# Gates of the second unit moved off GpSimd, last turns copied by ScalarE, one rounding in another form, and a new order

## The reference

```
mag = sqrt(a_re**2 + a_im**2); scale = min(mag, 0.999) / (mag + 1e-6)
ar, ai = a_re * scale, a_im * scale
S_re, S_im = ar*S_re - ai*S_im + outer(k, v), ar*S_im + ai*S_re
y[t] = q[t] @ S_re
```

## Time and profile before

| | |
|---|---|
| median of 3 runs | 913.99 us (913.25 to 916.9) |
| profiled execution, its own time | 915.01 us |
| its span | 913.3 us |
| mean granted TensorE clock | 0.987 |
| TensorE busy | 842.6 us, 92% |
| VectorE busy | 446.1 us, 49% |
| ScalarE busy | 490.1 us, 54% |
| GpSimd busy | 334.9 us, 37% |

### The profile page before, as it was taken

The page is one execution under the profiler, slowest core; times in us unless marked ns, Lnnn a source line. Parts: engine busy times, 40 slices in busy tenths (PEclk is TensorE's granted clock), DMA queues, the critical chain, the costliest instruction groups (busy, mean ns, idle before and its releaser), DMA issues.

```text
span 913.3 us, 14419 instructions
## 1 busy us (share of the span) xinstructions
PE 842.6 (92%) x5692; PEld 729.8 (80%) x5692; DVE 446.1 (49%) x628; ACT 490.1 (54%) x737; POOL 334.9 (37%) x254
## 2 busy tenths in 40 slices
PE   0168889889999999999999999999999999999997
PEld 0158889878887888788888888888888889898986
DVE  5689886848585848484848422333121121212020
ACT  7669778585959586868695535642121211211121
POOL 1165734534444444344444323556122221303120
PEclk9988999999999999999999999999999999999999
DMA  7664262444444443444352433021010101000000
GB/s 296 150 224 133 58 207 80 152 136 128 111 119 141 124 122 108 142 123 123 107 159 71 141 135 144 0 67 55 18 53 9 61 1 70 1 35 1 36 0 35
DMA packets 71011, 88.45 MB, mean 97 GB/s; under 512 B 15392, under 2 KB 55840, under 8 KB 70432
## 3 DMA queue, kind: packets, MB, share of 16 engines
q1 hardware_dynamic: 70944, 87.53, 30.8%
HBM read 59.13 MB, written 28.39 MB: 96 GB/s over the span
## 4 chain that ended last, share of the span: by engine, by line
PE 56%; issue 3%; POOL 1%; POOLq 0%; DVE 0%; ACT 0%
PE bank L1243 55%; POOL hl L593 1%; PE bank L1258 0%; POOLq L114 0%; DVE xl L947 0%; ACT osb L704 0%; POOLq L690 0%
## 5 line engine op out<-in xcount | busy, mean ns | idle before, releaser
L593 POOL TENSOR_TENSOR gl<-ge,gh 128x512 fp32r<-128x512 f32 x96 | 131.2, 1367 | 190.4 <-ACT gh L704 190.4
L947 DVE TENSOR_TENSOR hm<-bank,hm 128x512 f32<-128x512 f32 x72 | 49.8, 692 | 226.6 <-PE bank L1243 224.7
L1243 PE MATMUL bank<-xh,wih 128*128 128x512 f32 (+1 forms) x336 | 125.8, 374 | 6.9 <-DVE ge L944 3.6
L944 DVE SCALAR_TENSOR_TENSOR ge<-ge,bank 128x512 f32<-128x512 f32 x96 | 65.8, 685 | 130.9 <-ACT ge L704 130.9
L1243 PE MATMUL bank<-xh,wal 128*128 128x512 f32 x324 | 126.1, 389 | 0.0
L1243 PE MATMUL bank<-xl,wah 128*128 128x512 f32 x324 | 126.1, 389 | 0.0
L1243 PE MATMUL bank<-xh,wah 128*128 128x512 f32 x324 | 126.0, 389 | 0.0
L1243 PE MATMUL bank<-gh,woh 128*128 128x512 f32 (+1 forms) x336 | 124.1, 369 | 0.2
L1243 PE MATMUL bank<-xh,wil 128*128 128x512 f32 (+1 forms) x336 | 122.0, 363 | 0.0
L593 POOL TENSOR_TENSOR hl<-hm,hh 128x512 fp32r<-128x512 f32 x36 | 46.5, 1293 | 205.8 <-ACT hh L704 205.8
L1243 PE MATMUL bank<-xl,wih 128*128 128x512 f32 (+1 forms) x336 | 121.8, 363 | 0.0
(11 more groups left out here) (86 smaller groups left out, 1610.3 us busy)
## 6 DMA issues: line engine op xcount, KB each, us to landing
q_cols<-qp SPq DMA_DIRECT2D x24, 384.0 KB, 2.9
k_cols<-kp SPq DMA_DIRECT2D x24, 384.0 KB, 3.0
qt<-q_cols SPq DMA_DIRECT2D x24, 384.0 KB, 4.0
kt<-k_cols SPq DMA_DIRECT2D x24, 384.0 KB, 3.9
vv<-in_v SPq DMA_DIRECT2D x12, 448.0 KB, 4.6
qd<-in_q SPq DMA_DIRECT2D x12, 384.0 KB, 4.5
kd<-in_k SPq DMA_DIRECT2D x12, 384.0 KB, 5.2
x_rows<-x2s SPq DMA_DIRECT2D x6, 768.0 KB, 4.9
```

The costliest lines, as they stand in the source:

```text
L593: return nc.gpsimd.tensor_tensor(dst, whole, high.bitcast(f32), ALU.subtract)
L944: return nc.vector.scalar_tensor_tensor(out=dst, in0=a, scalar=s, in1=b, op0=op0, op1=op1)
L947: return nc.vector.tensor_tensor(dst, a, b, op)
L1243: return nc.tensor.matmul(dst, lhsT, rhs, start=start, stop=stop)
```

## The change

- `square_im`, `tangent` and `decayed` of unit 1 run on VectorE, as those of unit 0 do. `SOLO` is the count of parts that do; the semaphores `sq_im1`, `tan1` and `qkd1` now count through part 2.
- The copy of the last turns moves from VectorE (`reduced`) to ScalarE (`sines`, behind the first sine), and the next operation waits for it there.
- `reduced` of parts 3 and later rounds by a `scalar_tensor_tensor` whose second input is a broadcast [128, 1] tile `magic`. It used to be a `tensor_scalar` with two constants. `magic` is filled by one more memset on GpSimd, so the count of constants goes from 5 to 6.
- The tables of positions change. The diff has them all.

```diff
-        "signed": -8, "tangent": -11, "arctan": -10, "angle": -8, "scan_lam": -10, "center": -10, "exps": -7, "ends": -8,
-        "scan_phi": -7, "reduced": -6, "decayed_a": -9, "decayed_b": -8, ...
+        "signed": -8, "tangent": -12, "arctan": -10, "angle": -8, "scan_lam": -10, "center": -10, "exps": -7, "ends": -9,
+        "scan_phi": -7, "reduced": -6, "decayed_a": -9, "decayed_b": -7, ...
...
     AT_FIRST = {
-        "square": -49, "square_im": -49, "squared": -48, "root": -46, "denominator": -44, "inverse": -42, "log_decay": -39,
+        "square": -49, "square_im": -49, "squared": -49, "root": -47, "denominator": -44, "inverse": -40, "log_decay": -43,
...
-        "rotate_q_b": -26, "rotate_k_b": -24, "state_decay": -13, "s_a": -6, "s_b": 2, "kr_a": -3, "kr_b": 5, "masked_a": -2,
+        "rotate_q_b": -27, "rotate_k_b": -27, "state_decay": -12, "s_a": -6, "s_b": 1, "kr_a": -3, "kr_b": 4, "masked_a": -7,
...
-        "load_a": -50, "load_q": -48, "load_k": -45, "load_v": -46, "store_q_a": -27, "load_qt_a": -24, "store_k_a": -27,
+        "load_a": -50, "load_q": -48, "load_k": -45, "load_v": -46, "store_q_a": -29, "load_qt_a": -26, "store_k_a": -27,
...
     AT_SECOND = {
-        "square": -39, "square_im": -37, "squared": -39, "root": -35, "denominator": -34, "inverse": -30, "log_decay": -31,
-        "signed": -27, "tangent": -28, "arctan": -29, "angle": -22, "scan_lam": -28, "center": -24, "exps": -27, "ends": -26,
-        "scan_phi": -22, "reduced": -18, "decayed_a": -28, "decayed_b": -14, "sines": -16, "rotate_q_a": -13, "rotate_k_a": -12,
-        "rotate_q_b": -2, "rotate_k_b": -7, ...
+        "square": -39, "square_im": -42, "squared": -39, "root": -35, "denominator": -34, "inverse": -30, "log_decay": -31,
+        "signed": -24, "tangent": -30, "arctan": -29, "angle": -22, "scan_lam": -30, "center": -22, "exps": -27, "ends": -26,
+        "scan_phi": -22, "reduced": -18, "decayed_a": -21, "decayed_b": -21, "sines": -16, "rotate_q_a": -17, "rotate_k_a": -12,
+        "rotate_q_b": -2, "rotate_k_b": -10, ...
     SPLIT = {
-        "w_in_high": (-4, 9, 11, 20), "w_out_high": (-10, 8, 16, 25), "w_in_low": (1, 14, 16, 27), "w_out_low": (-6, 2, 13, 28),
-        "w_load": (-44, -43, -20, -8),
+        "w_in_high": (-4, 9, 11, 20), "w_out_high": (-3, 8, 16, 25), "w_in_low": (5, 14, 16, 26), "w_out_low": (-8, 2, 11, 29),
+        "w_load": (-44, -42, -20, -6),
...
+        SOLO = last_part(1) + 1
         def of_gate(eng, first, later, p):
-            if p < PAIR:
+            if p < SOLO:
...
# GpSimd                      now_later: unit 1's positions are left out too
-                    return now(what) and x != AT_FIRST[what] and x != AT_FIRST_B.get(what)
+                    return now(what) and x not in (AT_FIRST[what], AT_FIRST_B.get(what), STEPS + AT_SECOND[what])
# ScalarE, sines
                 if unit_of_part(p) < NU - UPC:
+                    func(of_part(last_turn[:, unit_of_part(p) % UPC], p).rearrange("p e j -> p (e j)"), slices(g.t1)[:, :, P - 1],
+                         ACT.Copy).then_inc(lst, 1)
                     act.wait_ge(lst, p + 1)
# VectorE, reduced
-                ts(g.t2, g.t3, 4.0 * MAGIC, ALU.add, 4.0 * MAGIC, ALU.subtract).then_inc(turn, 1)
+                if p <= PAIR:
+                    ts(g.t2, g.t3, 4.0 * MAGIC, ALU.add, 4.0 * MAGIC, ALU.subtract).then_inc(turn, 1)
+                else:
+                    stt(flat(g.t2), flat(g.t3), 4.0 * MAGIC, magic[:, 0:1].to_broadcast([P, PAIR * W]), ALU.add,
+                        ALU.subtract).then_inc(turn, 1)
...
-                u = unit_of_part(p)
-                if u < NU - UPC:
-                    dve.wait_ge(rr, p + 1)
-                    nc.vector.tensor_copy(of_part(last_turn[:, u % UPC], p)..., slices(g.t1)[:, :, P - 1]).then_inc(lst, 1)
# VectorE                     now_first: unit 1's positions are taken in
-                    return x in (AT_FIRST[what], AT_FIRST_B.get(what))
+                    return x in (AT_FIRST[what], AT_FIRST_B.get(what), STEPS + AT_SECOND[what])
```

More of the change, by code:

```diff
@@ L56, in build @@
         "square": -21, "square_im": -22, "squared": -20, "root": -17, "denominator": -17, "inverse": -13, "log_decay": -13,
-        "signed": -8, "tangent": -11, "arctan": -10, "angle": -8, "scan_lam": -10, "center": -10, "exps": -7, "ends": -8,
-        "scan_phi": -7, "reduced": -6, "decayed_a": -9, "decayed_b": -8, "sines": -4, "rotate_q_a": -4, "rotate_k_a": -2,
+        "signed": -8, "tangent": -12, "arctan": -10, "angle": -8, "scan_lam": -10, "center": -10, "exps": -7, "ends": -9,
+        "scan_phi": -7, "reduced": -6, "decayed_a": -9, "decayed_b": -7, "sines": -4, "rotate_q_a": -4, "rotate_k_a": -2,
         "rotate_q_b": 1, "rotate_k_b": 5, "state_decay": 3, "s_a": 6, "s_b": 10, "kr_a": 7, "kr_b": 11, "masked_a": 6,
         "masked_b": 10, "kr_evac_a": 7, "kr_evac_b": 11, "state_decayed_a": 6, "state_decayed_b": 8, "y_a": 8, "y_b": 11,
-        "inc_a": 10, "inc_b": 15, "state_add_a": 10, "state_add_b": 15, "x_high_a": 9, "x_low_a": 9, "x_high_b": 12,
+        "inc_a": 10, "inc_b": 16, "state_add_a": 10, "state_add_b": 15, "x_high_a": 8, "x_low_a": 9, "x_high_b": 12,
         "x_low_b": 12, "load_a": -22, "load_q": -7, "load_k": -7, "load_v": 7, "store_q_a": -3, "load_qt_a": -1,
@@ L67, in build @@
     AT_FIRST = {
-        "square": -49, "square_im": -49, "squared": -48, "root": -46, "denominator": -44, "inverse": -42, "log_decay": -39,
-        "signed": -36, "tangent": -40, "arctan": -38, "angle": -34, "scan_lam": -38, "center": -37, "exps": -34, "ends": -28,
-        "scan_phi": -34, "reduced": -33, "decayed_a": -33, "decayed_b": -32, "sines": -31, "rotate_q_a": -28, "rotate_k_a": -26,
-        "rotate_q_b": -26, "rotate_k_b": -24, "state_decay": -13, "s_a": -6, "s_b": 2, "kr_a": -3, "kr_b": 5, "masked_a": -2,
@@ new lines, in build @@
+        "signed": -36, "tangent": -40, "arctan": -38, "angle": -36, "scan_lam": -38, "center": -37, "exps": -34, "ends": -29,
+        "scan_phi": -34, "reduced": -33, "decayed_a": -33, "decayed_b": -31, "sines": -31, "rotate_q_a": -28, "rotate_k_a": -27,
+        "rotate_q_b": -27, "rotate_k_b": -27, "state_decay": -12, "s_a": -6, "s_b": 1, "kr_a": -3, "kr_b": 4, "masked_a": -7,
+        "masked_b": 1, "kr_evac_a": -1, "kr_evac_b": 2, "state_decayed_a": -21, "state_decayed_b": -13, "y_a": -3, "y_b": 4,
@@ L77, in build @@
+        "inc_a": 0, "inc_b": 4, "state_add_a": -1, "state_add_b": 5, "x_high_a": 0, "x_low_a": -1, "x_high_b": 3, "x_low_b": 5,
+        "load_a": -50, "load_q": -48, "load_k": -45, "load_v": -46, "store_q_a": -29, "load_qt_a": -26, "store_k_a": -27,
+        "load_kt_a": -24, "store_q_b": -25, "load_qt_b": -23, "store_k_b": -24, "load_kt_b": -22, "store_ends": -22,
+        "load_ends": -12, "tile": -2, "negative": -40, "small": -42,
     }
     AT_FIRST_B = {
-        "square": -48, "square_im": -48, "squared": -47, "root": -44, "denominator": -40, "inverse": -40, "log_decay": -36,
@@ L81, in build @@
-        "signed": -35, "tangent": -38, "arctan": -36, "angle": -33, "scan_lam": -36, "center": -34, "exps": -32, "ends": -27,
-        "scan_phi": -33, "reduced": -29, "sines": -30, "load_a": -49, "negative": -40, "small": -38,
+        "square": -47, "square_im": -48, "squared": -47, "root": -45, "denominator": -43, "inverse": -39, "log_decay": -37,
+        "signed": -35, "tangent": -39, "arctan": -36, "angle": -33, "scan_lam": -36, "center": -34, "exps": -33, "ends": -27,
+        "scan_phi": -32, "reduced": -29, "sines": -30, "load_a": -49, "negative": -37, "small": -38,
@@ L129, in build @@
         halfpi = sb("halfpi", [P, 1])
+        magic = sb("magic", [P, 1])
         tmp = ExitStack()
@@ L304, in of_part @@
             return t[:, p:p + 1] if p < PAIR else t[:, :]
+        SOLO = last_part(1) + 1
         def of_gate(eng, first, later, p):
-            if p < PAIR:
+            if p < SOLO:
                 eng.wait_ge(first, p + 1)
             else:
-                eng.wait_ge(later, p - 1)
+                eng.wait_ge(later, p - SOLO + 1)
         def of_rows(eng, z):
-            if z < 2 * PAIR:
+            if z < 4 * PAIR:
                 eng.wait_ge(qkd1, z + 1)
             else:
-                eng.wait_ge(qkd, z - 2 * PAIR + 1)
+                eng.wait_ge(qkd, z - 4 * PAIR + 1)
         def gates_loaded(eng, p):
@@ L1347, in second @@
                 last.then_inc(down, 1)
[L1349 removed]
+            pe.wait_ge(cst, 6)
             def attention(x):
```

22 lines of the change are left out of this document (8 added, 14 removed).

## The result

| | before | after |
|---|---|---|
| median of 5 runs | 914.82 us (913.25 to 916.9) | 922.88 us (921.31 to 923.25) |
| profiled execution, its own time | 915.01 us | 922.45 us |
| its span | 913.3 us | 920.7 us |
| mean granted TensorE clock | 0.987 | 0.981 |
| TensorE busy | 842.6 us | 849.0 us |

The ratio is 1.0093 (95% interval 1.0073 to 1.0113): slower by 0.9%. The forecast was 913.0 us with a range up to 919.5 (the narrower one that stands beside it ended at 917), so it was wrong in sign and outside its range.

A forecast was written before the change was run, and what follows sets the result against it. TensorE, full from 190 to 860 us, was taken as the bound, so only waits before 190 could yield. Profile 915.0 - 0.7 - 0.3 = 914.0, as a median 913.0 us; own range 909.5 to 917, wider range 905.5 to 919.5.

The forecast's parts named there:

- the hand-followed chain up to 72 us: Start and unit 1: instruction times followed by engine, from first matmul at 36.0 to unit 2's squared magnitude done at 71.0.
- the scalar-tensor form waits for GpSimd: Rounding of later units: each takes 1.8 us, 0.4 more than now; with the copy gone, 0.4 less VectorE time per unit.
- 0.3 sooner for the stretch 72 to 190: Copies and rounding of later units together, with the moved weight halves: 0.3 us sooner.
- I take 0.7 sooner, the middle between the two orders of the turns: State at 72 us: 0.7 us sooner, between 2.2 sooner (weight ahead of GpSimd's instruction) and 0.7 later (behind it).
- (a): Opening's gain holds: rotations 3.3 us sooner, low clock near 71 gone, ELU wait halved; 7.6 us faster, 906.4; chance 0.33.
- Bounds 3 sooner (one wait goes) and 3 later: Limits put on the 0.3 us gain between 72 and 190 us, in either direction.
- After 190: nothing: Stretch after 190 us: no effect, since TensorE has 0.85 us of idle there in all.
- (b): Moved low halves of w_in delay VectorE: 2.5 us late at 72, 2.8 more at the ELU wait; 919.3; chance 0.16.
- (c): Scalar-tensor rounding runs at half speed with two SBUF inputs, 1.9 us for 0.95; end 2 us later, 915.0; chance 0.03.

The follow-up runs named there:

- e10: Kernel before with only the copy of last turns moved to ScalarE; 914.54 us, ratio 1.0006.
- e11: Changed kernel with the copies of last turns on VectorE again; 921.59 us, ratio 1.0066.
- e9: Kernel before with only the rounding of parts 3 and later as a scalar-tensor-tensor; 916.56 us, ratio 1.0031.
- e5: Changed kernel run again, unedited; median 921.34 us, ratio 1.0073; its profiled execution took 916.81 us.
- e4: Changed kernel with the rounding of all parts as a tensor-scalar again; 915.06 us, ratio 1.0021.
- e2: Changed kernel with the first low half of w_in at position -1 instead of 5, unit 1's first Q rotation moved to 0; 916.22 us, ratio 1.0043.
- e6: Changed kernel with 70 idle matmuls put on TensorE ahead of four of its waits; 917.28 us, ratio 1.0031.
- e7: Kernel before with idle matmuls: 30 ahead of the second half of batch 0's K transposes, 22 ahead of unit 1's scores; 918.07 us, ratio 1.0033.
- e13: Single further profile of the changed kernel, unedited; 921.95 us, span 920.2.
- e3: Changed kernel with the fourth low half of w_in at position 27 instead of 26, behind the fifth ELU; 919.35 us, ratio 1.0066.
- e1: Changed code with the position tables of the kernel before, except unit 1's square_im and decayed; 922.45 us, ratio 1.0087.

## Why the prediction was wrong

**Right, within about 1 us: the hand-followed chain up to 72 us.** First matmul 36.0 said, 36.45 measured; arctangent of unit 1 40.5, 41.41; masking 42.8, 43.52; K rows 50.6, 51.48; TensorE's wait for them some 5, 5.4; sines 53.3, 54.02; rotation of Q 56.2, 57.04; first low half of `w_in` 63.3 to 67.8, 64.18 to 68.94, in 4.76 us instead of 1.76; squared magnitude of unit 2 done 71.0, 72.00. The steps as such were right, and each came 0.5 to 1.1 us later than I had it. The opening gave less than I had priced: the rotations of unit 0 end at 30.05, 0.8 us sooner and not 1.1. And the squared magnitude of unit 1, which I had at 30.6, starts at 31.43, 0.4 us later than before: its square is done at 30.92, and 0.5 us pass before VectorE goes on with the result. The root, the table load and the arctangent inherit that 0.8.

**Right in the size, wrong in the sum: the scalar-tensor form waits for GpSimd.** I took 0.4 more for each; 1.58 against 1.18 at the first, and 0.4 at each of the nine others. But I called the sum nothing, since 0.86 for the copy went with it, and so the term "0.3 sooner for the stretch 72 to 190" had the wrong sign. The copies proved worth nothing that the runs can tell (e10, e11) and the form 2.6 us in the kernel before (e9; 2.3 as spans of e5 and e4, both without the fall at 82), and undoing it gives 6 us back in the changed kernel (e4). By the Trainium skill, "SBUF — State Buffer", section "SBUF: two separate sides", this was to be expected of two SBUF inputs, and now a row shows it for this form; the half speed of "Vector Engine (DVE) Microarchitecture Reference", section "Points that are easy to get wrong", was again not seen (0.94 at 71.06 for 768 elements).

**Failed, first: "I take 0.7 sooner, the middle between the two orders of the turns".** The order of the turns was not open: my own steps put GpSimd's instruction 0.7 us ahead of the low half of `w_in`, and that order came. A middle between a case that the steps exclude and one that they give is no forecast. By the steps alone it was 0.7 later. The four profiles of the changed kernel have 1.7, 0.4, 1.5 and 1.9 at the first ELU.

**Failed, second: nothing priced the clock on the slower side.** "Bounds 3 sooner (one wait goes) and 3 later" for 72 to 190 was worked out from VectorE's instructions. Measured was 5.36 at the sixth ELU and 5.09 at the 15th. I had the low clock as a gain in rival (a) and as a risk at the first MLP slice (there it was, for the first 13 of its 18 matmuls, 0.41 us each after the first, until 72.0), but did not carry the lateness on: the chain behind it brought unit 1's K rows 1.7 us late (81.14 against 79.45), TensorE's wait for them grew from 0.88 to 3.13, and behind it the third MLP slice ran at 1.2 GHz, 4.2 us instead of 2.4. e2 shows the first link, e6 and e7 the second. But the clock is only a part: it cost 1.8 us there in the profiles in which it fell for long, 0.2 in e13 and nothing in e5, which still is 2.27 late at the sixth ELU.

**Failed, third: "After 190: nothing".** From the 19th ELU on the changed kernel loses another 2.0 us in the first profile (5.37 to 7.4) and 0.9 in e5. Up to the last maximum it is 0.7, with 1.5 us of idle time on TensorE between 190 and 860 where there had been 0.85. The wait near the end (2.9 us for `hl`) stands ahead of low clock, in the kernel before too. In the last 21 us, from the last maximum to the end, the changed kernel lost 1.3 us that way in the first profile, and in e5 0.2.

**The rivals.** (b) named the place, the moved low half of `w_in`, and its test came true (first MLP slice after 68 us: 69.08). Its price of 919.3 was 3 us short of the profiled 922.45. The other half of it did not come: the fourth low half cost TensorE nothing (e3), and the longest ELU wait is 3.4 us and not over 5. So its sum was the nearest by other terms than its own, with the clock and the form of the rounding missing. It should have had more than 0.16. (c) had the sign of the form right and its mechanism wrong: turns at the port and not half speed. (a) had nothing: of the 3.3 us by which the rotations were to be sooner, 2.45 came, and the weight behind them took them back.

**Open.** What decides in one execution whether the clock falls behind a wait of 1.4 to 3.1 us: the same kernel did both. Why e4, which edits nothing ahead of 97 us, has so few long executions. It may be that they need both falls, at 82 and at 190, and e4 spares the second. The profiles of e1, e3 and e11 have both as well, with spans of 920.7, 921.9 and 920.3; but so has e10's, with 914.3, and single profiles are too few to say so. Why ten roundings, each 0.4 us longer, cost 2.6 us in one order and 6 in the other is open too, and so is what the one fall at 82 has to do with it, at 1.8 us.

## What to carry over

When a wait in front of TensorE grows from under 1 us to 2 or 3, do not price the wait alone: look at whether the trace's other waits stand ahead of a stretch at half clock, and price both cases, with the fall and without, since one kernel can show either. Follow the order of two engines at their shared port through by start times, and take the case that the steps give, not a middle. And where executions of one kernel fall into two groups, compare the groups: an edit can move the share of long executions and little else.

## What the runs showed of the chip

- One kernel, two profiles, the same wait (3.13 and 2.64 us): in one TensorE's granted clock went to 0.50 for the 6 us behind it, in the other it stayed at 1.00. Over sixteen profiles the clock fell at waits in this place as short as 1.37 us and stayed up over ones of up to 2.68.
- A busier TensorE sum is not by itself a later end: e9 has 847.1 us busy in a span of 913.7, e5 842.3 in 915.1. What a matmul at the low clock costs is seen only where TensorE has no wait behind it that takes it up.
- An idle float32 matmul of 128 by 128 by 128 leaves two records of some 0.12 us each in sequence at full clock (24 in 2.94 us), and with 12 of them in the wait the clock stayed up, where it fell in three of the four profiles without.
- A scalar-tensor-tensor behind a running GpSimd instruction: 2.44 us at 86.01, with GpSimd's 1.83 at 85.82; alone 0.94.
